# Both blocks of global scores behind the weighing of unit 0, and the first batch's second head lowered by the vector engine

## The reference, cut to what matters

```python
batch, n_heads, seq_l, seq_g, head_dim = (4, 8, 512, 32, 64)
k_all = concatenate([k_g, k_l]); v_all = concatenate([v_g, v_l])
out_g = softmax(scale * q_g @ k_all.T) @ v_all            # 32 global queries see all 544 keys
s_ll  = where(|i - j| <= 32, scale * q_l @ k_l.T, -1e9)   # 512 local queries: a window ...
s_lg  = scale * q_l @ k_g.T                               # ... and the 32 global keys
out_l = softmax([s_lg, s_ll]) @ [v_g, v_l]
x     = [out_g, out_l] of all heads                       # 4 * 544 = 2176 rows of 512
```

## Time and profile before

| | |
|---|---|
| median of three runs | 319.38 us (318.92 to 320.33) |
| the profiled execution | 318.87 us, its span 317.1 us |
| PE busy | 306.9 us, 97% |
| DVE busy | 211.9 us, 67% |
| ACT busy | 139.0 us, 44% |
| POOL busy | 64.8 us, 20% |
| chain that ended last | PE 86%, DVE 7%, issue 5% |

### The profile page before, as it was taken

The page is one execution under the profiler, slowest core; times in us unless marked ns, Lnnn a source line. Parts: engine busy times, 40 slices in busy tenths (PEclk is TensorE's granted clock), DMA queues, the critical chain, the costliest instruction groups (busy, mean ns, idle before and its releaser), DMA issues.

```text
span 317.1 us, 7840 instructions
## 1 busy us (share of the span) xinstructions
PE 306.9 (97%) x2987; PEld 220.3 (69%) x2987; DVE 211.9 (67%) x443; ACT 139.0 (44%) x293; POOL 64.8 (20%) x62
## 2 busy tenths in 40 slices
PE   7999999999999999999998999999999999999994
PEld 4576777777777786233335888788888888888883
DVE  3887988888889556721258877566556666566572
ACT  1366766666566642111137554432334222532531
POOL 0543434434335001000008964000000000000000
PEclk9999999999999999999999999999999999999999
DMA  7999999999999969999999000030003000300202
GB/s 236 376 375 341 334 377 407 370 401 372 375 390 343 391 232 378 414 407 412 415 419 406 21 2 0 1 132 2 0 0 134 0 0 0 135 1 0 99 2 74
DMA packets 18032, 69.56 MB, mean 219 GB/s; under 512 B 4176, under 2 KB 5840, under 8 KB 14288
## 3 DMA queue, kind: packets, MB, share of 16 engines
q1 hardware_dynamic: 18000, 69.14, 57.7%
HBM read 64.41 MB, written 4.46 MB: 217 GB/s over the span
## 4 chain that ended last, share of the span: by engine, by line
PE 86%; DVE 7%; issue 5%; ACT 1%; POOL 1%; DVEq 0%; POOLq 0%
PE ps L846 20%; PE ps L849 20%; PE ps L550 6%; PE ps L595 5%; PE ps L821 5%; PE ps L746 4%; PE ps L777 4%; PE ps L587 3%; PE ps L566 3%; DVE sc L1101 3%; PE ps L606 2%; PE ps L541 2%; PE ps L560 2%; PE ps L581 2%; PE ps L658 1%
## 5 line engine op out<-in xcount | busy, mean ns | idle before, releaser
L849 PE MATMUL ps<-wlo,gg 128*128 128x512 f32 x204 | 80.5, 395 | 0.0
L846 PE MATMUL ps<-whi,gg 128*128 128x512 f32 x204 | 80.3, 394 | 0.0
L1307 DVE SCALAR_TENSOR_TENSOR nt<-uu,ps 128x512 f32<-128x512 f32 (+2 forms) x80 | 48.4, 607 | 47.3 <-ACT uu L1008 47.1
L1008 ACT ACTIVATE uu<-ps 128x512 f32<-128x512 f32 (+2 forms) x80 | 42.8, 537 | 84.0 <-PE ps L821 78.2
L457 POOL TENSOR_TENSOR sc<-sc,mx 128x640 f32<-128x640 f32 x32 | 40.1, 1253 | 53.5 <-DVE mx L1106 53.5
L1318 DVE TENSOR_TENSOR gg<-nt,ps 128x512 fp32r<-128x512 f32 (+2 forms) x80 | 47.9, 601 | 0.1
L846 PEld LDWEIGHTS ps<-whi,gg 128*128 128x128 f32 x204 | 38.4, 188 | 8.8
L849 PEld LDWEIGHTS ps<-wlo,gg 128*128 128x128 f32 x204 | 38.4, 188 | 8.0
L1101 DVE TENSOR_TENSOR sc<-ps,cst 128x640 f32<-128x640 f32 x32 | 26.2, 820 | 7.5 <-PE ps L550 5.9
L821 PE MATMUL ps<-cT,Pst 128*128 128x512 f32 (+2 forms) x80 | 28.9, 361 | 0.7 <-DVE Pst L1289 0.6
L595 PEld LDWEIGHTS ps<-vv,eT 128*64 128x64 f32 x512 | 18.7, 137 | 13.4 <-issue 11.0
(11 more groups left out here) (130 smaller groups left out, 384.6 us busy)
## 6 DMA issues: line engine op xcount, KB each, us to landing
w<-moe_w SPq DMA_DIRECT2D x11, 2048.0 KB, 11.2
vv<-v_t SPq DMA_DIRECT2D x8, 1170.0 KB, 7.7
w<-moe_w SPq DMA_DIRECT2D x14, 512.0 KB, 11.6
kT<-k_t SPq DMA_DIRECT2D x16, 416.0 KB, 6.3
out<-oo SPq DMA_DIRECT2D x17, 256.0 KB, 2.2
qT<-q_t SPq DMA_DIRECT2D x16, 256.0 KB, 7.3
win<-moe_w_in SPq DMA_DIRECT2D x4, 1024.0 KB, 16.6
wout<-moe_w_out SPq DMA_DIRECT2D x3, 1024.0 KB, 22.2
```

The source lines that it names most:

```text
L846: pe.matmul(o, g, hi, start=(c == 0), stop=False)
L849: mm = pe.matmul(o, g, lo, start=False, stop=(c == NC - 1))
L1008: nc.scalar.activation(uu[c % 2][:, 0:width], cols(h_bank(i, c), width), ACT.Square, scale=(1.0 / 3) ** 0.5).then_inc(square_ready, 1)
L1307: nc.vector.scalar_tensor_tensor(out=nt[c % 2][:, 0:width], in0=uu[c % 2][:, 0:width], scalar=1.0, in1=cols(h_bank(i, c), width), op0=ALU. ...
```

## The change

Both blocks of global scores of a batch (units 4 and 9) are made together, behind the weighing of unit 0 of their own batch. The products of the two blocks alternate, and the second block's heads are put at other rows (`global_rows`), so that the eight products of 512 columns fall on eight different tiles of the array. `scg`, `gmx` and the banks of the second block are its own (banks 2 and 3). The scores of heads (4,5) go from behind unit 0 to behind unit 1, those of (6,7) from behind unit 2 to behind unit 3; those for the next batch stay behind units 5 and 7. DVE takes both global maxima at the start of unit 0, ahead of normalising it, and masks heads 4 to 7 behind units 1 to 4 (before: 0 to 3). `rank(k)` is the place of unit k's scores in the new order. The semaphores of the loads follow. In SP's list the keys and queries of pair 2 move ahead of the first weights, and keys and queries of pair 3 behind them. In the first batch the scores of unit 4 leave the part before the loop, and DVE subtracts the second head's maximum, after POOL has done the first head's.

```diff
@@ -118,9 +118,9 @@
         eT = [place(f"eT{n}", [P, 640], F32) for n in range(2)]
-        scg = place("scg", [P, SL + SG], F32)
+        scg = [place(f"scg{n}", [P, SL + SG], F32) for n in range(2)]
         mx = [place(f"mx{n}", [P, 4], F32) for n in range(2)]
-        gmx = place("gmx", [P, 2], F32)
+        gmx = [place(f"gmx{n}", [P, 2], F32) for n in range(2)]
         den = place("den", [P, 4], F32)
...
@@ -289,13 +290,19 @@
         def scores_ps(k):
-            return 0 if k in GQ else 2 * head_of(k)[1]
+            return 2 * (k // 5) if k in GQ else 2 * head_of(k)[1]
+        def rank(k):
+            return k if k < 5 else 5 if k == 9 else k + 1
+        def global_rows(qd, j):
+            return 32 * (j ^ qd)
...
         def probs_of(k):
-            return scg if k in GQ else pr[k % 2]
+            return scg[k // 5] if k in GQ else pr[k % 2]
@@ -317,23 +324,23 @@
         AHEAD = 5
-        SCORES_AT = {(u - AHEAD) % U: u for u in (0, 2, 4, 5, 7, 9)}
+        SCORES_AT = {5: 0, 7: 2, 0: 4, 1: 5, 3: 7}
...
-                sp.wait_ge(scores_ready, U * (i - 1) + GQ[pr // 2] + 1)
-                sp.dma_start(kT[pr][:], k_t[i - 1, pr]).then_inc(qk_loaded[pr], 16)
+                sp.wait_ge(scores_ready, U * (i - 1) + (6, 6, 8, 10)[pr])
+                sp.dma_start(kT[pr][:], k_t[i - 1, pr]).then_inc(qk_loaded[pr] if pr < 2 else global_loaded, 16)
...
-                sp.wait_ge(scores_ready, U * (i - 1) + (2, 4, 7, 9)[pr])
-                sp.dma_start(qT[pr][:], q_t[i - 1, pr]).then_inc(qk_loaded[pr], 16)
+                sp.wait_ge(scores_ready, U * (i - 1) + (2, 4, 8, 10)[pr])
+                sp.dma_start(qT[pr][:], q_t[i - 1, pr]).then_inc(qk_loaded[pr] if pr < 2 else q_loaded[pr], 16)
             def global_queries(i):
-                sp.wait_ge(scores_ready, U * i)
-                sp.dma_start(qgT[:], qg_t[i - 1]).then_inc(qg_loaded, 16)
+                sp.wait_ge(scores_ready, U * (i - 1) + 6)
+                sp.dma_start(qgT[:], qg_t[i - 1]).then_inc(global_loaded, 16)
@@ -352,8 +359,8 @@
             keys(1, 2)
+            keys(1, 3)
             queries(1, 2)
-            keys(1, 3)
             queries(1, 3)
@@ -363,7 +370,7 @@
                     sp.dma_start(x[SG * b:SG * b + SG, NT - 1, D * h:D * h + D],
-                                 xg[qd][32 * j:32 * j + 32, :]).then_inc(xg_spread[qd], 16)
+                                 xg[qd][global_rows(qd, j):global_rows(qd, j) + 32, :]).then_inc(xg_spread[qd], 16)
...
@@ -457,7 +464,7 @@
-            for k in range(4):
+            for k in (0, 2, 3):
                 lower(1, k)
@@ -517,29 +524,35 @@
                 if k in GQ:
-                    pe.wait_ge(qg_loaded, 16 * i)
-                    pe.wait_ge(masked_ready, U * i + k - 1)
+                    pe.wait_ge(global_loaded, 48 * i)
                 else:
-                    pe.wait_ge(qk_loaded[head_of(k)[0]], 32 * i)
-                    pe.wait_ge(masked_ready, U * i + k)
+                    pair = head_of(k)[0]
+                    pe.wait_ge(*((qk_loaded[pair], 32 * i) if pair < 2 else (q_loaded[pair], 16 * i)))
+                pe.wait_ge(masked_ready, U * i + rank(k))
...
             def scores(k):
-                bank = scores_ps(k)
                 if k in GQ:
-                    for part in range(2):
+                    def one(qd, j, part):
+                        pr = 2 * qd + j // 2
+                        r = slice(64 * (j % 2), 64 * (j % 2) + 64)
+                        own = kT[pr][r, 0:768].rearrange("r (b n) -> r b n", n=96)[:, :, 0:64]
+                        keys = kT[pr][r, 768:768 + SG] if part else own
+                        at = global_rows(qd, j)
+                        o = ps[at:at + 32, scores_ps(GQ[qd]) + part, 0:SG if part else 512]
+                        return pe.matmul(o, qgT[r, pr, :], keys, start=True, stop=True)
+                    for j in range(4):
+                        for qd in range(2):
+                            one(qd, j, 0)
+                    for qd in range(2):
                         for j in range(4):
-                            pr = 2 * (k // 5) + j // 2
-                            r = slice(64 * (j % 2), 64 * (j % 2) + 64)
-                            own = kT[pr][r, 0:768].rearrange("r (b n) -> r b n", n=96)[:, :, 0:64]
-                            keys = kT[pr][r, 768:768 + SG] if part else own
-                            o = ps[32 * j:32 * j + 32, bank + part, 0:SG if part else 512]
-                            mm = pe.matmul(o, qgT[r, pr, :], keys, start=True, stop=True)
-                    mm.then_inc(scores_ready, 1)
+                            mm = one(qd, j, 1)
+                        mm.then_inc(scores_ready, 1)
                 else:
@@ -579,7 +592,7 @@
                             mm = pe.matmul(ps[32 * j:32 * j + 32, 6 + k % 2, 0:D + 1],
-                                           et[:, P * c + 32 * j:P * c + 32 * j + 32], ve[qd][:, j, c, :],
+                                           et[:, P * c + 32 * j:P * c + 32 * j + 32], ve[qd][:, j ^ qd, c, :],
                                            start=(c == 0), stop=(c == 4))
@@ -610,12 +623,12 @@
                     u = SCORES_AT.get(k)
-                    if last and u is not None and u < AHEAD:
+                    if last and k >= AHEAD:
                         u = None
...
                         if u is not None:
-                            wait_scores(i + (u < AHEAD), u)
+                            wait_scores(i + (k >= AHEAD), u)
@@ -635,8 +648,6 @@
             turn_probs(1, 0)
-            wake_for_scores(1, 4, cst)
-            scores(4)
             with pe.Fori(1, NB) as i:
@@ -912,7 +923,7 @@
                     nc.scalar.activation(e[:], e[:], ACT.Exp,
-                                         bias=gmx[:, 1:2], scale=SCALE).then_inc(exp_ready, 1)
+                                         bias=gmx[k // 5][:, 1:2], scale=SCALE).then_inc(exp_ready, 1)
                 else:
@@ -1083,28 +1094,31 @@
-            def maxima(i, k):
-                dve.wait_ge(scores_ready, U * i + k + 1)
-                h = head_of(k)[2]
-                if k in GQ:
-                    dve.wait_ge(probsT_ready, U * i + k - 4)
+            def global_maxima(i):
+                for qd in range(2):
+                    k = GQ[qd]
+                    dve.wait_ge(scores_ready, U * i + rank(k) + 1)
+                    dve.wait_ge(probsT_ready, U * (i - 1) + k + 1)
                     dve.sem_inc(passed_by_dve, 1)
                     nc.vector.tensor_tensor_reduce(
-                        scg[:], cols(scores_ps(k), SL + SG), cst[:, C_ZERO:C_ZERO + 1].broadcast_to([P, SL + SG]),
-                        1.0, -3.0e38, ALU.add, ALU.max, gmx[:, 0:1]).then_inc(masked_ready, 1)
-                    dve.wait_ge(masked_ready, U * i + k + 1)
-                    nc.vector.tensor_scalar(gmx[:, 1:2], gmx[:, 0:1], -SCALE, None, ALU.mult).then_inc(gmax_ready, 1)
-                else:
-                    dve.wait_ge(exp_ready, U * i + (unit_of(h - 2) if h >= 2 else unit_of(h + 6) - U) + 1)
-                    bank = scores_ps(k)
-                    nc.vector.tensor_tensor(sc[h % 2][:].rearrange("p (b n) -> p b n", b=2),
-                                            ps[:, bank:bank + 2, 0:320],
-                                            cst[:, C_MASK:C_MASK + 640].rearrange("p (b n) -> p b n", b=2),
-                                            ALU.add).then_inc(masked_ready, 1)
-                    dve.wait_ge(masked_ready, U * i + k + 1)
-                    nc.vector.tensor_reduce(mx[h % 2][:], sc[h % 2][:].rearrange("p (j n) -> p j n", j=4),
-                                            AX.X, ALU.max).then_inc(max_ready, 1)
+                        scg[qd][:], cols(scores_ps(k), SL + SG), cst[:, C_ZERO:C_ZERO + 1].broadcast_to([P, SL + SG]),
+                        1.0, -3.0e38, ALU.add, ALU.max, gmx[qd][:, 0:1]).then_inc(masked_ready, 1)
+                for qd in range(2):
+                    dve.wait_ge(masked_ready, U * i + rank(GQ[qd]) + 1)
+                    nc.vector.tensor_scalar(gmx[qd][:, 1:2], gmx[qd][:, 0:1], -SCALE, None, ALU.mult).then_inc(gmax_ready, 1)
+            def maxima(i, k):
+                dve.wait_ge(scores_ready, U * i + rank(k) + 1)
+                h = head_of(k)[2]
+                dve.wait_ge(exp_ready, U * i + (unit_of(h - 2) if h >= 2 else unit_of(h + 6) - U) + 1)
+                bank = scores_ps(k)
+                nc.vector.tensor_tensor(sc[h % 2][:].rearrange("p (b n) -> p b n", b=2),
+                                        ps[:, bank:bank + 2, 0:320],
+                                        cst[:, C_MASK:C_MASK + 640].rearrange("p (b n) -> p b n", b=2),
+                                        ALU.add).then_inc(masked_ready, 1)
+                dve.wait_ge(masked_ready, U * i + rank(k) + 1)
+                nc.vector.tensor_reduce(mx[h % 2][:], sc[h % 2][:].rearrange("p (j n) -> p j n", j=4),
```

(33 more changed lines are left out.)

## The result

Ten runs of the changed kernel have a median of 321.48 us (320.58 to 322.76), beside 319.26 us for the kernel before on the same chips. The ratio is 1.0076, 95% interval 1.0058 to 1.0094: 1.9 to 3.0 us slower. The predicted time was 322.5. The profiled execution took 322.44 us (span 320.5), near the top of its runs; the profiled one of before took 318.87 (span 317.1).

A forecast was written before the change was run, and what follows sets the result against it. The prediction took PE's chain of waits, not loads, to bound the attention. Batch 4 starting 0.48 us late plus 3.02 in the last batch gave 318.87 + 3.5 = 322.4, stated as 322.5 us, range 317.4 to 325.4.

The forecast's parts named there:

- the walk: Step-by-step timing of one batch through PE, DVE, POOL and ACT: 25.41 us instead of 24.91, 0.50 slower.
- the last batch: With no further scores to hide stalls behind, it takes 22.50 us instead of 19.48: 3.02 slower.
- the sum: Batch 4 starts 0.48 us late, the last batch loses 3.02: 318.87 + 3.5 = 322.4 us, given as 322.5.
- Fewer passes on PE: Joint block of global scores 1.22 us instead of 2.10 (bounds 1.05 and 2.10), 0.88 less PE work a batch.
- S1: S(k) is when PE starts the turning ahead of weighing unit k, from S(0) = 0; S1 was put at 3.07 us.
- rival 3: The eight products don't run together: block stays 2.10 us, 0.88 more in each of four batches, 325.9 us; chance 0.10.
- The global maxima on DVE: DVE waits some 1.4 us for the joint block; then two maxima and two scalings precede normalising unit 0: a loss.
- The long way: From unit k+1's mask on DVE through POOL, ACT's exponentials and copies to the earliest S(k): 4.77 us, hidden before.
- Rival 2: The stall behind mask 6, ahead of S5, does not come as POOL and ACT answer sooner: 318.4 us, no change; chance 0.20.
- The start: S1 of batch 1 at 17.02 us instead of 17.73, 0.71 earlier; DVE's 0.82 us subtraction is hidden.
- Waits of SP: Load issues waiting in SP's list: no cost; next keys wanted some 12 us after S1 and land in 6.3.
- rival 4: A load comes late by a microsecond a batch, since DMA is full: 326 us; chance 0.03.

The follow-up runs named there:

- same_tiles: Changed kernel with both global blocks' heads at the same rows, so their products fall on four tiles instead of eight: 324.18 us, ratio 1.0168.
- norm_first: Changed kernel with unit 0 normalised ahead of the two global maxima instead of behind them: 321.97 us, ratio 1.0086.
- behind9: Changed kernel with the joint block behind unit 9 of the batch before, and the pairs behind units 0 and 2 as in the kernel before: 319.48 us, ratio 1.002.
- after_short: Changed kernel with POOL subtracting the maxima from only 8 of 160 columns for units 6, 7 and 8: 321.4 us, ratio 1.0078.
- before_short: Kernel before, with POOL subtracting the maxima from only 8 of 160 columns for units 6, 7 and 8: 318.94 us, ratio 0.9993.
- values_up_short: Changed kernel with queries of pairs 2 and 3 loaded behind the next batch's values, and POOL subtracting 8 of 160 columns for units 6 to 8: 318.83 us, ratio 0.999.
- old_loads: Changed kernel with SP's loads in the order of the kernel before everywhere, the first batch included: 321.81 us, ratio 1.0092.
- w1_first: Changed kernel with the 2 MB weight w1 loaded ahead of the loads of pairs 2 and 3 in the loop: 322.66 us, ratio 1.0127.
- before_dve_lowers: Kernel before, with DVE instead of POOL subtracting the second head's maximum in the first batch: 319.12 us, ratio 1.0007.
- w1_first_short: Changed kernel with w1 loaded ahead of pairs 2 and 3, and POOL subtracting only 8 of 160 columns for units 6 to 8: 321.45 us, ratio 1.0075.
- pool_lowers: Changed kernel with POOL instead of DVE subtracting the second head's maximum in the first batch: 323.01 us, ratio 1.0127.

## Why the prediction was right

It was right: slower, 321.5 for 322.5, and the stalls of the walk are found in the trace, place by place. That the last batch and the sum came out so close is luck in good part, as shown below. By its steps:

- *Fewer passes on PE.* 1.08 for the predicted 1.22, which is the lower bound's 1.05 but for 0.03: the second block's short products cost next to nothing. A slip stands in the sum: 1.75 + 1.22 is 2.97, not the 3.07 taken for S1; measured is 2.83. With same_tiles beside it, rival 3 is out. The rule of the Trainium skill (TensorEngine Tiling (Array Packing), Restrictions and Gotchas) that different row tiles can't use one PSUM bank at once isn't borne out for different partitions: products of both row halves go to one bank here, and eight ran together.
- *The global maxima on DVE.* DVE idles 1.68 us ahead of the first (1.4 predicted). It begins 0.45 us after S1, where the walk took the 0.21 of a mask. The two errors cancel: the first maximum comes at 67.68, S0 + 3.28, to the hundredth as forecast, and what the block saved over the forecast never reached DVE. From the first to the second is 0.65, not 0.77. norm_first and behind9 bear out that the place of the block costs, and not the order behind it.
- *The walk.* Relative to S0 the trace has S2 6.23, S4 11.34, S5 13.61, next S0 24.98, where the prediction has 6.35, 11.68, 14.07 and 25.41. The 0.12 of S2 is that between the maxima. From there to normalising unit 0 (69.20, S0 + 4.80, for 5.14) another 0.22 is saved at the scalings, and these 0.34 are the whole of S4's difference; S5 has 0.12 more from the long way. So the batch is 0.07 longer than before and not 0.50. The new stall ahead of S5 is 0.86 (78.01 less 75.74 and 1.41); 0.98 was said. The long way is 78.01 - 73.36 = 4.65 for 4.77.
- *Rival 2*, that this stall doesn't come, is out. In after_short this stall goes with POOL's 1.25 us, so these are on the path in a batch now; in before_short nothing changed. What POOL costs in the whole time is not shown, since after_short is no faster and values_up_short changes the loads too.
- *The last batch.* 112.13 - 89.38 = 22.75 for 22.50, with S5 to S8 within 0.3 of the walk (14.07, 16.67, 19.27, 21.00). This is where the loss is: 3.27 us more than 19.48, while the start and batches 1 to 3 together are 0.32 shorter (89.38 for 89.70). But the agreement is luck. In the traces with little or nothing of the two other waits this batch took 21.73 (old_loads) and 21.94 (w1_first), 2.3 to 2.5 more than before, so the walk's own stalls make some 0.8 less than the 3.02 forecast. The rest, 0.8 to 1.0 us, is what the walk had put at nothing: the late vg transfers, which make S1 3.39 for the 2.83 of batch 3, and the 0.52 ahead of S4, which passes over DVE's mask of unit 8 to S7 (19.27, and 18.46 in w1_first).
- *What the 0.52 is* stays open. In the changed kernel's trace the exponentials of unit 5 had ended at 100.17 and the copies of unit 4 at 100.79, PE itself was free at 101.35. A packet of 16 KB on the queue that the page calls "instruction" ended at 100.47, 1.40 us ahead of that turning. Seven traces have such a wait there, of 0.26 to 1.09 us, and in all of them the turning follows the end of that packet by 1.28 to 1.51 us. Where the packet ended early enough (98.02 in w1_first, 100.09 in old_loads) there is no wait. So it may be PE's own instructions that came late; no run tested it.
- *The start.* S1 of batch 1 at 16.91 for 17.02. DVE's subtraction took 0.83 us from 11.40, and mask 2 came at 12.26: hidden, as forecast.
- *Waits of SP.* This step was wrong: "No cost". It set 12 us against 6.3 for keys. The values, wanted at once when a batch begins, were not looked at. In the kernel before, the last vg of batch 4 landed 9.1 us after its issue at 80.5, some 0.6 ahead of its use, so there was hardly any slack; with the 0.5 MB of queries ahead of them vv landed 10.5 us after its issue instead of 8.0, and the last vg 11.3. How much of that is the queries' doing is not shown: with the old order (old_loads) vv took 9.4. In the changed kernel it shows as 0.46 us at the start of batch 4 (from L594 to L547 3.14 us, 2.68 in the batch ahead of it), and in after_short 0.92. That is rival 4 in small: it comes in one batch of four, not in each.

Why the sum came out so close: batches 2 and 3 were predicted 0.4 too long each, and the last began 0.8 earlier than forecast (89.38 for 90.18). The last batch was 0.25 longer, and the work behind the attention 0.45 longer, in part a wait for a weight that the prediction took as moving along with the rest. By medians the kernel is 2.2 us slower, by the interval 1.9 to 3.0, and by the profiled pair 3.6; the walk's 3.5 was worked out for such a pair, and the profiled run after lies near the top of its ten. The sum has a slip too: a profiled run of 322.4 that lies 0.5 below the median means 322.9 for the median, not 322.5; measured is 321.48. So the way and the mechanism were forecast, and the loss of the median runs was 1.3 us less than the walk's.

## What to carry to other kernels

Work saved on the busiest engine counts only if the chain that feeds it keeps its lead. Before moving a producer later, follow its results through every queue to the place where the busiest engine needs them, and look at the last turn of the loop, where no later work hides anything. When DMA is full, check the load with the least time to spare, not the one that the edit names, and of its parts the one issued last. And a forecast that agrees for a stretch is worth splitting: here stalls that were set too long and two waits that were left out made the last batch agree.

## What the runs showed of the hardware

Eight products of 64 by 32 tiles (two row halves, four column groups, 512 columns of f32) ran at once in the time of four: 1.08 us for a joint block, 2.00 when both blocks share four tiles. And with the DMA engines full, the same 1.17 MB load for batch 4 landed 7.2 to 9.7 us after its issue with 4.3 MB of its batch issued ahead of it (7.2 in before_dve_lowers, 8.0 in the kernel before, 9.4 in old_loads, 9.7 in values_up_short), and 8.8 to 11.0 us with 4.8 MB ahead (8.8 in same_tiles, 9.4 in w1_first_short, 10.1 in w1_first, 10.5 in the changed kernel, 11.0 in pool_lowers). The two ranges overlap, so the bytes ahead don't set it alone. Where PE waited, it was for the last of four transfers of 32.5 KB issued right behind it: 11.3 us under way in the changed kernel, 12.0 in w1_first_short. By medians, kernels that differ only in such a list lie up to 1.2 us apart (321.48, 321.81, 322.66), and up to 2.6 us with the shorter way (318.83, 321.4, 321.45).
